# Moving a product of the output weights with a DFT table to the start of a fused attention, gate and FFT kernel

## The reference

```
state = alpha[t][:, None] * state + outer(k[t], v[t]);  x[t] = q[t] @ state      # per head
gate = sigmoid(sum over 5 taps of conv_w[k] * x shifted by 4 - k tokens)
y = (gate * (x @ w_val)) @ w_out
u = y + real(fft over features (fft over tokens (y)))
out = u + relu(layernorm(u) @ w_ch1) @ w_ch2
```

## Time and profile before

| what | value |
|---|---|
| median of three runs | 550.34 us (549.83 to 550.49) |
| the profiled execution's own time | 550.07 us |
| its span, first to last instruction | 548.2 us |
| TensorE busy | 541.3 us, 99% of the span |
| VectorE busy | 397.9 us, 73% |
| ScalarE busy | 207.5 us, 38% |
| granted TensorE clock | 1.00 of full speed |

### The profile page before, as it was taken

How to read it: one execution, slowest core, us unless ns; L and a number is a source line. 1 busy time by engine, 2 the same in 40 slices (tenths; PEclk the granted TensorE clock), 3 DMA queues, 4 the chain that set the end, 5 groups by cost and what they waited for, 6 DMA issues and landing times.

```text
span 548.2 us, 13474 instructions
## 1 busy us (share of the span) xinstructions
PE 541.3 (99%) x5547; PEld 519.6 (95%) x5547; DVE 397.9 (73%) x874; ACT 207.5 (38%) x487; POOL 12.9 (2%) x29
## 2 busy tenths in 40 slices
PE   8999999999999999999999999999999999999997
PEld 7989999999999999999999999999999999999997
DVE  8998889999858786989767486998936484653322
ACT  5655554424352135325262134325244134322221
POOL 0010000000000000000000000000000000000000
PEclk9999999999999999999999999999999999999999
DMA  8778212354212010455322001256200000022000
GB/s 265 235 273 303 49 31 66 111 170 125 72 50 78 30 44 24 132 144 169 96 62 68 29 1 45 85 141 197 78 8 23 30 1 1 1 59 83 13 22 30
DMA packets 36301, 47.21 MB, mean 86 GB/s; under 512 B 11632, under 2 KB 25200, under 8 KB 35984
## 3 DMA queue, kind: packets, MB, share of 16 engines
q1 hardware_dynamic: 34080, 40.97, 25.3%
q0 software_dynamic: 1728, 5.11, 2.7%
q10 hardware_dynamic: 432, 0.27, 0.2%
HBM read 35.32 MB, written 11.01 MB: 85 GB/s over the span
## 4 chain that ended last, share of the span: by engine, by line
PE 94%; DVE 3%; issue 1%; ACT 1%; DVEq 0%; POOL 0%; POOLq 0%
PE bank L1077 45%; PE bank L1166 28%; PE evens L1104 5%; PE bank L1151 4%; PE bank L1146 2%; PE bank L1234 2%; PE bank L1197 2%; PE sums L1128 2%; PE bank L1268 1%; PE bank L1173 1%; PE bank L1203 1%; DVE w_lo L1000 1%; PE bank L1278 1%; PE sums L1113 1%; ACT un L662 0%
## 5 line engine op out<-in xcount | busy, mean ns | idle before, releaser
L1059 DVE SCALAR_TENSOR_TENSOR h_lo<-bank,h_hi 128x256 fp32r<-128x256 f32 x144 | 60.2, 419 | 94.1 <-ACT h_hi L796 89.7
L1077 PE MATMUL bank<-unT_hi,w_hi 128*128 128x256 f32 x432 | 123.8, 287 | 0.9 <-DVE h_lo L1059 0.6
L1077 PE MATMUL bank<-unT_lo,w_hi 128*128 128x256 f32 x432 | 122.1, 283 | 0.0
L796 ACT ACTIVATE h_hi<-bank 128x256 fp32r<-128x256 f32 x144 | 54.9, 381 | 177.4 <-PE bank L1077 177.3
L1077 PE MATMUL bank<-unT_hi,w_lo 128*128 128x256 f32 x432 | 121.4, 281 | 0.0
L1166 PE MATMUL bank<-w_hi,h_hi 128*128 128x384 f32 x288 | 98.8, 343 | 0.0
L1166 PE MATMUL bank<-w_lo,h_hi 128*128 128x384 f32 x288 | 97.6, 339 | 0.0
L1166 PE MATMUL bank<-w_hi,h_lo 128*128 128x384 f32 x288 | 97.3, 338 | 0.0
L1077 PEld LDWEIGHTS bank<-unT_hi,w_hi 128*128 128x128 f32 x432 | 81.2, 188 | 4.2 <-DVE h_lo L1059 1.9
L1077 PEld LDWEIGHTS bank<-unT_hi,w_lo 128*128 128x128 f32 x432 | 81.6, 189 | 0.0
L1077 PEld LDWEIGHTS bank<-unT_lo,w_hi 128*128 128x128 f32 x432 | 81.5, 189 | 0.0
(11 more groups left out here) (189 smaller groups left out, 960.2 us busy)
## 6 DMA issues: line engine op xcount, KB each, us to landing
v_in<-in_v_dram SPq DMA_DIRECT2D x24, 224.0 KB, 3.1
w_raw<-in_w_dram SPq DMA_DIRECT2D x2, 2304.0 KB, 10.7
a_in<-in_alpha_dram SPq DMA_DIRECT2D x44, 96.9 KB, 2.3
q_in<-in_q_dram SPq DMA_DIRECT2D x44, 96.0 KB, 2.2
k_in<-in_k_dram SPq DMA_DIRECT2D x44, 96.0 KB, 2.3
turned_blocks<-turned SPq DMA_DIRECT2D x15, 256.0 KB, 2.3
kdT<-turned_blocks SPq DMA_DIRECT2D x60, 64.0 KB, 2.0
out_dram<-u POOLq DMA_DIRECT2D x18, 192.0 KB, 2.3
```

The costliest lines, as they stand in the source:

```text
L796: act.activation(h_hi[:, f % HBUF, :], ps[:, 0:GW], ACT.Relu).then_inc(s_hi, 1)
L1059: dve.scalar_tensor_tensor(h_lo[:, f % HBUF, :], ps[:, 0:GW], 0.0, h_hi[:, f % HBUF, :].bitcast(F32), ALU.max, ALU.subtract).then_inc(s_re ...
L1077: last = pe.matmul(ps, l, r, start=(i == 0), stop=(i == len(mms) - 1))
```

## The change

Five edits. (1) SP issues the loads of `dftd` and `woutT` right behind chunk 1's loads, and no longer beside chunks 3 and 4. (2) The first third of the product, `wd` 0, stands where the four identity products (`idle`) stood, behind chunk 0's `state`; its `wdl` stands in `LATE[0]`, behind `tapj` 0. Both leave `LATE[3]`. (3) The first `xlo` goes from `LATE[3]` to `LATE[4]`. (4) `tap_blocks` gives two blocks for c = 3 as well: TensorE does the taps of block 1 there. (5) VectorE's and ScalarE's set for block 1 covers tokens 512 to 767 where it covered 384 to 767, and `GATES` names ranges where it named halves.

```
-TAP_SETS = ((K - 1, 0, HALF), (K - 1, HALF, HALF + 2 * CH), (1, HALF, S), (K - 1, HALF + 2 * CH, S))
-GATES = ((K - 1, 0, 0), (1, 1, 2), (K - 1, 1, 3))
+TAP_SETS = ((K - 1, 0, HALF), (K - 1, HALF, HALF + 2 * CH), (1, 4 * CH, S), (K - 1, HALF + 2 * CH, S))
+GATES = ((K - 1, 0, HALF, 0), (1, 4 * CH, S, 2), (K - 1, HALF, S, 3))
...
-LATE = {0: [("tapj", 0, 0, 0), ("odd", 0, 0, 0)], 1: [("tapj", 0, 1, 0)], 2: [("tapj", 0, 2, 0), ("whi", 0, 0, 0), *x_parts("xhi", 0)],
-        3: [("wd", 0, 0, 0), ("tapj", 0, 3, 0), ("wdl", 0, 0, 0), ("tapv", 0, 0, 1), ("xlo", 0, 0, 0), ("tapv", 0, 0, 2)],
-        4: [("wd", 0, 1, 0), ("tapj", 0, 4, 0), ("wdl", 0, 1, 0), ("tapv", 0, 0, 3), ("wlo", 0, 0, 0), ("tapv", 0, 0, 4)]
+LATE = {0: [("tapj", 0, 0, 0), ("wdl", 0, 0, 0), ("odd", 0, 0, 0)], 1: [("tapj", 0, 1, 0)], 2: [("tapj", 0, 2, 0), ("whi", 0, 0, 0), *x_parts("xhi", 0)],
+        3: [("tapj", 0, 3, 0), ("tapv", 0, 0, 1), ("tapv", 0, 0, 2)],
+        4: [("wd", 0, 1, 0), ("tapj", 0, 4, 0), ("wdl", 0, 1, 0), ("xlo", 0, 0, 0), ("tapv", 0, 0, 3), ("wlo", 0, 0, 0), ("tapv", 0, 0, 4)]
...
         if c == 0:
-            sch += [("idle", 0, 0, 4)]
+            sch += [("wd", 0, 0, 0)]
...
-            return TAP_BLOCKS[c >= NCH // 2]
+            return TAP_BLOCKS[c >= 4]
...
-            beside = {2: ("wval",), 3: ("dft",), 4: ("woutT",), 5: ("wout", "w1", "w2")}
+            beside = {1: ("dft", "woutT"), 2: ("wval",), 5: ("wout", "w1", "w2")}
...
-                    m, half, last_set = GATES[a]
+                    m, first, end, last_set = GATES[a]
...
-                    g = gate[:, m, half * HALF:(half + 1) * HALF]
+                    g = gate[:, m, first:end]
...
-                        for i, (m, half, _) in enumerate(GATES):
-                            if (m, half) == (a, f):
+                        for i, (m, first, end, _) in enumerate(GATES):
+                            if m == a and first < (f + 1) * HALF and end > f * HALF:
                                 dve.wait_ge(s_sig, i + 1)
```

## The result

The changed kernel takes 551.04 us (median of 18 runs, 550.73 to 553.02), the kernel before 550.28 us (18 runs). The ratio is 1.0021, with a 95% interval of 1.0014 to 1.0027: the change makes the kernel slower by 0.8 to 1.5 us. The medians differ by 0.76 us, the low end of that. The forecast was 551.9 us in a range of 550.2 to 553.7, slower. The profiled execution has a span of 549.1 us against 548.2.

The account below looks back on a forecast made before the run. The prediction took TensorE to bound the prologue from 12.93 us on. Product delay 2.33, `wdl` 0.18, removed work -1.02 and mask 0.10 sum to +1.6 us: 550.34 + 1.6 = 551.9 us, range 550.2 to 553.7.

Parts of the forecast that it names:

- TensorE bounds the prologue: From 12.93 us to the first value product at 47.55, each microsecond of TensorE work added or removed moves the end equally.
- The removed work, 1.02 us: In chunk 3 TensorE does two tap blocks, 2.23 us, in place of 3.25 us of work: 1.02 us gained.
- The mask of chunk 5, 0.1 us: VectorE's mask ends at 41.78 us, `y` of chunk 5 would want it at 41.70: 0.1 us charged.
- VectorE's saved taps, 0: In chunk 5's list, 504 ns of VectorE's taps saved, counted as 0 gain.
- The delay at the product, 2.33 us: In chunk 0, tables land at about 13.1 us, so `wd` 0 waits and `scores` of chunk 1 begins 2.33 us late.
- `wdl` at 0.18: In `LATE[0]`, the moved `wdl` 0 costs its 0.18 us again.
- case of data in time: Rival at chunk 0's product: tables land by 12.6 us, delay 0.86 to 1.8, sum +0.1 to +1.1 us; chance 0.27.
- the forecast's own 551.4 to 553.6: Main case at chunk 0's product: tables land between 12.6 and 14.8 us, time 551.4 to 553.6, likeliest 551.9; chance 0.50.
- The delay made up again: Rival in chunks 1 to 3: the delay is caught up before chunk 4, leaving -0.7 to -1.2 us; chance 0.10.
- The clock falls: Rival from `wd` 0 to `tapj` 0: TensorE slows after resting, up to 2.8 us more, about 554.7 us; chance 0.08.
- Chunk 2's alpha, 0: Queued behind the tables, it lands at about 13.6 us, but its scan ends before the delayed `scores`: 0.
- ScalarE's two copies, 0: Copies of `wd` 0 to `wd_hi` and `wd_lo`, in ScalarE's idle time and ahead of chunk 1's `xT` copy: 0.

Follow-up runs that it names:

- Experiment 4: The kernel before with the tap edits alone (two tap blocks on TensorE in chunk 3, shorter set on VectorE and ScalarE): 551.82 us, ratio 1.0032.
- Experiment 3: The changed kernel, but the taps of block 1 in chunk 3 stay on VectorE: 551.23 us, ratio 1.0030 to the kernel before.
- 11: The changed kernel with 22 warming products instead of 18: 551.97 us, ratio 1.0046 to the kernel before.
- 1: The changed kernel, but the moved product multiplies stand-in data and waits for no load: 550.23 us, ratio 1.0005 to the kernel before.
- 12: The kernel before with 22 warming products instead of 18: 551.08 us, ratio 1.0022.
- 10: The changed kernel, but SP issues the two tables beside chunk 2, at about 9.6 us instead of 4.6: 558.0 us, ratio 1.0141 to the kernel before.
- Experiment 8: The kernel before with the early loads of the two tables alone: 550.24 us, ratio 1.0004.
- 7: The kernel before with 16 warming products instead of 18: 549.79 us, ratio 0.9996.
- 9: The changed kernel with tables before chunk 1's q and k, block 1's chunk 3 taps on VectorE, first xlo and two VectorE taps later, 16 warming products: 549.78 us.
- 6: The changed kernel with tables ahead of chunk 1's q and k, block 1's chunk 3 taps on VectorE, first xlo in chunk 5's list: 550.61 us, ratio 1.0007.

## Why the prediction was right, point by point

**TensorE bounds the prologue: right, with one limit.** Experiment 4 puts 1.12 us on TensorE in chunk 3 and gets at least that back as time. Experiment 3 shows the limit: take more than about 1 us off TensorE there and VectorE's list, from the mask of chunk 3 to that of chunk 5, becomes the chain.

**The removed work, 1.02 us: right.** The chain of the kernel before has at the same places:

```profile
30.75 1.09 PE evens L1104 x16
...
37.68 1.09 PE evens L1104 x16
...
43.01 0.87 PE bank L1151 x32
```

`scores` of chunk 4 to `scores` of chunk 5 takes 38.79 - 32.85 = 5.94 us after, 37.68 - 30.75 = 6.93 before: 0.99 us gained. **The mask of chunk 5, 0.1 us: right.** `y`'s second part takes 1.02 us where it took 0.87, 0.15 us of waiting. The timeline after names what for:

```profile
44.06 0.80 PEld L1151 LDWEIGHTS bank<-scores,v_in 128*32 128x32 f32 x32 [0.21 <-DVE scores L961]
```

0.11 us come back at the third `wdl`, which takes 0.30 instead of 0.41; the forecast did not have that.

**VectorE's saved taps, 0: right as far as shown.** Experiment 4 gives none of them back.

**The delay at the product, 2.33 us: the term that was mis-sized.** It measured 1.99 us between the profiles. The tables' landing sets it, however early TensorE comes: from the end of `y` of chunk 0 in the profile before, 11.73 us, it is a wait of 0.97 us to 12.70, and a product of 2.22 us in a hole of 1.20, 1.02 us more. The forecast had 1.47 and 0.86. So the wait was put 0.50 us too long: the tables landed at 12.66 us and not at 13.1. The count of bytes was good; the lag behind the last byte was taken from k (1.85 us), and it was 1.4. Where the landing comes differs from one execution to the next, though: in the six profiles that issue the tables as the change does it runs from 12.4 (11) to 13.5 us (3), and 13.1 lies inside. And the product was put 0.16 us too short: 1.96 us is its step in chunk 3, behind `kt`, while behind `scores` it takes 2.15 (39.88 us in the chain above) and behind `y` without a wait 2.15 as well (1). With `wdl` at 0.18 as forecast, the sum of the terms as measured is 1.99 - 0.07 (`scores` and `kt` themselves) + 0.18 - 0.99 + 0.15 - 0.11 = 1.15 us, which is what the chain shows at 48.71 and 69.35 us, and what the ratio says. The forecast was 1.6. Some luck is in that agreement. `scores` of chunk 0 came at 7.78 us in the profile before and at 8.44 in the one after. Had it come at 8.44 in both, less of the wait would be left, and the same sum would give 1.15 - 0.66 = 0.49 us, by estimate. The difference of the medians, 0.76 us, lies between the two.

**What of it is the wait, and what the length.** The median without the wait (1) lies 0.14 us above before, where the prediction's case of data in time had +0.1; the change lies 0.76 above. By the ratios it is 0.3 against 1.2 us, with intervals that just meet at 1.0014. So the wait is most of the loss, and the product's own length is paid by the shorter chunk 3, as the sum had it. The split varies: the time at which `scores` of chunk 0 starts ran from 7.3 to 8.8 us in the profiles with 18 warming products. The prediction did not see this variation.

**The rivals.** Data in time, or nearly: nearer than forecast. The tables landed 0.06 us behind the 12.6 us that bound this case, and 551.04 us lies in its span of 550.4 to 551.4, and below the forecast's own 551.4 to 553.6. The sign, the wait and the parts of the sum are the forecast's; its likeliest size is not. Whether the loss is over 0.2%, where the prediction drew the line to no change, the interval (0.14 to 0.27%) leaves open. The delay made up again: no; chunks 1 to 3 still take 5.9 us each (26.94 - 21.02 = 5.92 in the changed kernel). The clock falls: in the median no, in single executions yes. Of the 18 executions of the change one, of 553.02 us, has a mean clock of 0.997, as has the 553.62 us execution of 3, whose profile shows the fall at the product, and the 554.68 us one of 11. For the change itself that the fall is at the same place is inferred from this. None of the 77 executions of the kernel before that were timed beside experiments 1 to 12 is under 0.999. The prediction set the price at 2.8 us and the condition at "a wait well over the one I expect"; a rest of 1.33 us was enough in 3, and the product alone lost 1.7 us by it. So it asked for too long a wait. That a wait for loads ahead of products costs the full clock is what the Trainium skill says in "TensorE: Matmul & The Clock Gate", section "HAM oscillation"; the traces of 3 and 10 agree, with 0.50 granted, and in 3 the wait was shorter than those of the page's example.

**Chunk 2's alpha, 0: right in the change, by cover alone.** Experiment 8 shows 1.14 us of waiting for it once `scores` of chunk 1 is early. **ScalarE's two copies, 0:** no wait for them shows in the chain, and no experiment took them apart.

No version was shown to beat the kernel before: 7 and 9 lie 0.3 and 0.1 us below it, inside their intervals. 7 and 9 are faster than the change, since their intervals end at 1.0005 and 1.0007 where that of the change begins at 1.0014.

## What to carry to other kernels

Before filling a hole in an engine with real work, ask for two things: that the work is no longer than the hole, and that its operands land before the hole opens, counted in bytes behind everything already in the queue. Work that waits in the filler's place turns a free hole into a stall for all that follows it on the engine, and moving its load forward only moves the wait to another load. Filler products may also hold the clock, which no run here shows for certain: look at single executions and their clocks, not at the median alone.

## What the runs showed of the hardware that was not expected

- The warming products took a different time in each execution, at a granted clock that reads 1.00 throughout: with 18 of them `scores` of chunk 0 began between 7.31 and 8.76 us, with 16 at 7.46 and 8.19, with 22 at 8.52 and 8.96. The mean duration of their 36 matmul records ran from 330 ns (8) to 394 ns (1). The kernel before spreads by 1.3 to 2.1 us in its groups of runs, and this start alone is about as much.
- A rest of 1.33 us in front of the product was followed by a granted clock of 0.50 from 14 to 17 us (3). In the profiled change a rest of 0.31 us was not, and neither was the hole of 0.70 us in front of `scores` in 6. What TensorE did ahead of the rest was the same in 3 and in the change: a wait of 0.78 us for ScalarE before `sum`, then `sum` and `y`.
- Whichever of tables and k of chunk 1 stands last in the queue lands between 12.4 and 13.5 us (nine profiles).
